# One attention stage, another order: queues of all five engines rearranged within a pair of heads

## The reference

```python
q_bits = (np.einsum('bhsd,dk->bhsk', q, proj) > 0)      # the same for k; 6 bits give a bucket
mask = q_bucket[:, :, :, None] == k_bucket[:, :, None, :]
scores = np.where(mask, scale * np.matmul(q, k.transpose(0, 1, 3, 2)), -1000000000.0)
attn = np.exp(scores - np.max(scores, axis=-1, keepdims=True))
attn = attn / (np.sum(attn, axis=-1, keepdims=True) + 1e-09)
x = np.matmul(attn, v)                                   # reshaped to 1536 x 512
...
h = np.maximum(x @ w_in, 0.0)                            # 512 x 2048
x = h * h @ w_out                                        # 2048 x 512
...
h = np.maximum(x[mask] @ w1[e], 0.0)                     # 8 experts, 192 tokens each
out[mask] = h @ w2[e]
```

## Time and profile before

| | us |
|---|---|
| median of 3 runs | 838.34 (834.74 to 838.97) |
| profiled execution, its own time | 838.97 |
| its span in the trace | 837.2 |
| PE busy over the span | 783.4 (94%) |
| ACT, DVE, POOL busy | 377.2, 379.8, 398.9 |

### The profile page before, as it was taken

How to read it: one execution, slowest core, us unless ns; L and a number is a source line. 1 busy time by engine, 2 the same in 40 slices (tenths; PEclk the granted TensorE clock), 3 DMA queues, 4 the chain that set the end, 5 groups by cost and what they waited for, 6 DMA issues and landing times. The chain is left out here.

```text
span 837.2 us, 14217 instructions
## 1 busy us (share of the span) xinstructions
PE 783.4 (94%) x4720; PEld 714.6 (85%) x4720; DVE 379.8 (45%) x875; ACT 377.2 (45%) x655; POOL 398.9 (48%) x326
## 2 busy tenths in 40 slices
PE   5999999999999799999999999984599999999986
PEld 3898898898887688999999999973499999999986
DVE  6576576576672443322232234224555345345500
ACT  2677777777676455545545554530012122212221
POOL 5567777777577576646656675640100110011001
PEclk9999999999999899999999999995599999999999
DMA  6564775875541000100000010010635455364541
GB/s 157 121 150 109 157 180 127 187 187 126 141 126 51 0 1 0 38 1 0 1 38 0 0 39 0 0 38 0 220 122 173 166 176 183 119 218 149 179 170 38
DMA packets 43687, 81.38 MB, mean 97 GB/s; under 512 B 17176, under 2 KB 17176, under 8 KB 43136
## 3 DMA queue, kind: packets, MB, share of 16 engines
q1 hardware_dynamic: 41440, 74.58, 31.5%
q0 software_dynamic: 2048, 6.29, 2.3%
q10 hardware_dynamic: 160, 0.00, 0.0%
HBM read 54.55 MB, written 6.29 MB: 73 GB/s over the span
## 5 line engine op out<-in xcount | busy, mean ns | idle before, releaser
L1122 PE MATMUL banks<-xt_hi,split_parts 128*128 128x384 f32 (+1 forms) x512 | 142.2, 339 | 0.2 <-POOL split_parts L886 0.2
L309 POOL TENSOR_TENSOR pt_lo<-pt,pt_hi 128x768 fp32r<-128x768 f32 x64 | 117.7, 1846 | 48.0 <-ACT pt_hi L438 38.4
L1133 PE MATMUL banks<-split_parts,h_hi 128*128 128x512 f32 x384 | 122.8, 401 | 5.7 <-DVE h_lo L1048 5.6
L886 POOL TENSOR_TENSOR split_parts<-w_in_sb,split_parts 128x512 fp32r<-128x512 f32 x64 | 84.4, 1319 | 91.1 <-ACT split_parts L879 89.8
L1045 DVE TENSOR_TENSOR h<-relu 128x384 f32<-128x384 f32 x64 | 43.6, 681 | 184.6 <-ACT relu L1000 184.6
L431 ACT ACTIVATE pt<-banks 128x768 f32<-128x768 f32 x96 | 78.1, 813 | 60.8 <-PE banks L683 54.2
L544 DVE TENSOR_REDUCE mx<-banks 128x1 f32<-128x768 f32 x96 | 90.5, 957 | 23.4 <-PE banks L710 19.5
L1566 PE MATMUL banks<-x_cols,w_in_sb 128*128 128x192 f32 x512 | 96.6, 342 | 1.1 <-ACT x_cols L1346 1.1
L1122 PEld LDWEIGHTS banks<-xt_hi,split_parts 128*128 128x128 f32 x512 | 94.3, 190 | 3.3 <-POOL split_parts L886 0.5
L1580 PE MATMUL banks<-expert_hidden,w_out_sb 128*128 128x192 f32 x512 | 94.0, 334 | 0.0
L890 POOL TENSOR_TENSOR split_parts<-w_out_sb,split_parts 128x512 fp32r<-128x512 f32 x64 | 84.2, 1315 | 16.2 <-ACT split_parts L882 16.2
(11 more groups left out here) (195 smaller groups left out, 1354.6 us busy)
## 6 DMA issues: line engine op xcount, KB each, us to landing
w_in_sb<-in_moe_w SPq DMA_DIRECT2D x8, 2048.0 KB, 9.7
w_out_sb<-in_moe_w SPq DMA_DIRECT2D x8, 2048.0 KB, 8.6
w_in_sb<-in_moe_w_in SPq DMA_DIRECT2D x8, 512.0 KB, 6.5
w_out_sb<-in_moe_w_out SPq DMA_DIRECT2D x8, 512.0 KB, 6.4
w_out_sb<-in_k SPq DMA_DIRECT2D x16, 192.0 KB, 3.7
w_out_sb<-in_q SPq DMA_DIRECT2D x16, 192.0 KB, 4.0
v_raw<-in_v SPq DMA_DIRECT2D x16, 192.0 KB, 3.4
ka<-split_parts SPq DMA_DIRECT2D x16, 192.0 KB, 3.0
```

Source lines behind the costliest of these rows:

```text
L309: pool.tensor_tensor(pt_lo[x % 2][:], pt[j % 2][:], pt_hi[x % 2][:].bitcast(fp32), ALU.subtract).then_inc(los, 1)
L886: pool.tensor_tensor(wil[i], in_view(f), wih[i].bitcast(fp32), ALU.subtract).then_inc(wils, 1)
L1122: last = pe.matmul(PB[i][:, 0:HALF], w_[:, k, :], x_[:, xs], start=n == 0, stop=n == 3 * DT - 1)
L1133: last = pe.matmul(PB[2 + t][:], h_[:, tc], w_[:], start=start and n == 0, stop=stop and n == 2, skip_group_check=True)
```

## The change

No instruction is added or removed. Within a pair the lists of all engines are written in another order:

- PE: a pair begins with `z_k` and tile 0, then `weigh_low(2p - 1, 4)` and `weigh(2p - 1, 5)`, then tile 1 and `z_q`. In the odd head tile 0 comes before `weigh_low(2p, 4)`, tile 1 before the first two score tiles of the next head, and `weigh_low(2p + 1, 1)` before tile 4. Some `fallback`, `weigh_high` and `weigh_low` change places.
- ACT: `high(p - 1)` moves up to just behind `expo(2p, 0)`, `k_high` moves down behind `expo_high(2p, 1)`, `q_high` up ahead of `row`, `v_high` down behind `row` and `v_sum_high`.
- POOL: `low(p - 1)` and `k_low(p + 2)` exchange places.
- DVE: `k_bits` before `q_bits`, `max_done` before `sum_v` or the last `row_max` before `sum_v`.
- SP: `free_row(2p - 1)` first; both `weights` and `more_q` move into the second half of the pair.

```diff
--- before.py
+++ after.py
@@ -244,24 +244,25 @@
             more_k(2)
             more_q(2)
             for p in range(PAIRS):
+                if p:
+                    free_row(2 * p - 1, 1)
                 asm_kb(2 * p + 1, 1)
                 part_ka(1, p % 2)
-                if p:
-                    free_row(2 * p - 1, 1)
                 asm_qb(2 * p + 1, 1)
                 if p:
                     load_v(2 * p + 1, 1)
-                weights(2 * p)
                 part_qa(1, p % 2)
-                weights(2 * p + 1)
                 if p + 1 < PAIRS:
                     asm_kb(2 * p + 2, 0)
                     asm_qb(2 * p + 2, 0)
                     free_row(2 * p, 0)
+                more_q(p + 3)
+                weights(2 * p)
+                if p + 1 < PAIRS:
+                    load_v(2 * p + 2, 0)
                     part_ka(0, (p + 1) % 2)
-                    load_v(2 * p + 2, 0)
                 more_k(p + 3)
-                more_q(p + 3)
+                weights(2 * p + 1)
                 if p + 1 < PAIRS:
                     part_qa(0, (p + 1) % 2)
             for loaded in (ka_in, kb_in, qa_in, qb_in):
@@ -346,8 +347,8 @@
             k_low(pool, 1)
             q_low(pool, 1)
             for p in range(PAIRS):
-                if p + 2 < PAIRS:
-                    k_low(pool, p + 2)
+                if p:
+                    low(p - 1)
                 low_part(2 * p, 1)
                 low_part(2 * p, 2)
                 low_part(2 * p, 3)
@@ -355,8 +356,7 @@
                 v_low_part(2 * p + 1, 1)
                 if p + 2 < PAIRS:
                     q_low(pool, p + 2)
-                if p:
-                    low(p - 1)
+                    k_low(pool, p + 2)
                 low_part(2 * p + 1, 1)
                 low_part(2 * p + 1, 2)
                 low_part(2 * p + 1, 3)
@@ -466,10 +466,11 @@
             v_sum_high(0)
             for p in range(PAIRS):
                 expo(2 * p, 0)
+                high(p - 1)
                 sums(2 * p - 1, 1)
-                k_high(p + 2)
                 expo(2 * p, 1)
                 expo_high(2 * p, 1)
+                k_high(p + 2)
                 expo(2 * p, 2)
                 expo_high(2 * p, 2)
                 expo(2 * p, 3)
@@ -484,13 +485,12 @@
                     split["in_high"](act, 0, 0)
                     split["in_high"](act, 1, 1)
                     split["out_high"](act, 0, 0)
-                v_high(2 * p + 1, 1)
                 expo_high(2 * p, 4)
                 expo(2 * p, 5)
-                high(p - 1)
+                q_high(p + 2)
                 row(2 * p + 1, 1)
-                q_high(p + 2)
                 v_sum_high(2 * p + 1)
+                v_high(2 * p + 1, 1)
                 expo(2 * p + 1, 0)
                 sums(2 * p, 0)
                 expo(2 * p + 1, 1)
@@ -502,9 +502,9 @@
                 expo(2 * p + 1, 4)
                 expo_high(2 * p + 1, 4)
                 expo(2 * p + 1, 5)
+                v_sum_high(2 * p + 2)
                 row(2 * p + 2, 0)
                 v_high(2 * p + 2, 0)
-                v_sum_high(2 * p + 2)
             sums(HEADS - 1, 1)
             high(PAIRS - 1)
 
@@ -593,15 +593,15 @@
                     turn(2 * p - 1, 1, 0)
                     turn(2 * p - 1, 1, 1)
                 if not last:
+                    k_bits(p + 1, kbit[w]).then_inc(kbits, 1)
                     q_bits(p + 1, qbit[w]).then_inc(qbits, 1)
-                    k_bits(p + 1, kbit[w]).then_inc(kbits, 1)
                 row_max(2 * p + 1, 0)
                 row_max(2 * p + 1, 1)
                 row_max(2 * p + 1, 2)
                 row_max(2 * p + 1, 3)
                 row_max(2 * p + 1, 4)
+                row_max(2 * p + 1, 5)
                 sum_v(2 * p + 1, 1)
-                row_max(2 * p + 1, 5)
                 max_done(2 * p + 1)
                 v_low(2 * p + 1, 1)
                 turn(2 * p, 0, 0)
@@ -613,8 +613,8 @@
                     row_max(2 * p + 2, 3)
                     row_max(2 * p + 2, 4)
                     row_max(2 * p + 2, 5)
+                    max_done(2 * p + 2)
                     sum_v(2 * p + 2, 0)
-                    max_done(2 * p + 2)
                 invert(p)
                 if not last:
                     v_low(2 * p + 2, 0)
@@ -761,15 +761,15 @@
 
             def pair(p, w, first, last):
 
-                if not first:
-                    weigh(2 * p - 1, 1, 5)
+                if not last:
+                    z_k(p + 1, w)
                 scores_t(2 * p, 0, p, 0)
                 if not first:
-                    weigh_low(2 * p - 1, 1, 4, False, True)
+                    weigh_low(2 * p - 1, 1, 4)
+                    weigh(2 * p - 1, 1, 5, False, True)
+                scores_t(2 * p, 0, p, 1)
                 if not last:
                     z_q(p + 1, w)
-                    z_k(p + 1, w)
-                scores_t(2 * p, 0, p, 1)
                 weigh(2 * p, 0, 0, True)
                 scores(2 * p + 1, 1, p, 0, None if last else p + 1)
                 scores_t(2 * p, 0, p, 2)
@@ -777,11 +777,11 @@
                 weigh_high(2 * p, 0, 1)
                 scores(2 * p + 1, 1, p, 2, None if last else p + 1)
                 scores_t(2 * p, 0, p, 3)
+                fallback(2 * p, 0, 0)
                 scores(2 * p + 1, 1, p, 3, None if last else p + 1)
-                fallback(2 * p, 0, 0)
                 weigh_low(2 * p, 0, 1)
+                fallback(2 * p, 0, 1)
                 scores(2 * p + 1, 1, p, 4, None if last else p + 1)
-                fallback(2 * p, 0, 1)
                 scores_t(2 * p, 0, p, 4)
                 scores(2 * p + 1, 1, p, 5, None if last else p + 1)
                 weigh_high(2 * p, 0, 2)
@@ -791,13 +791,13 @@
                 weigh_low(2 * p, 0, 3)
                 rows(2 * p + 1, 1)
                 weigh(2 * p, 0, 5)
+                scores_t(2 * p + 1, 1, p, 0)
                 weigh_low(2 * p, 0, 4)
-                scores_t(2 * p + 1, 1, p, 0)
                 weigh_high(2 * p, 0, 4, False, True)
+                scores_t(2 * p + 1, 1, p, 1)
                 if not last:
                     scores(2 * p + 2, 0, p + 1, 0, None)
                     scores(2 * p + 2, 0, p + 1, 1, None)
-                scores_t(2 * p + 1, 1, p, 1)
                 weigh(2 * p + 1, 1, 0, True)
                 scores_t(2 * p + 1, 1, p, 2)
                 if not last:
@@ -811,17 +811,17 @@
                 weigh_high(2 * p + 1, 1, 2)
                 if not last:
                     scores(2 * p + 2, 0, p + 1, 5, None)
+                weigh_low(2 * p + 1, 1, 1)
+                scores_t(2 * p + 1, 1, p, 4)
                 fallback(2 * p + 1, 1, 0)
-                scores_t(2 * p + 1, 1, p, 4)
-                weigh_low(2 * p + 1, 1, 1)
+                weigh_high(2 * p + 1, 1, 3)
                 weigh_low(2 * p + 1, 1, 2)
                 fallback(2 * p + 1, 1, 1)
-                weigh_high(2 * p + 1, 1, 3)
                 scores_t(2 * p + 1, 1, p, 5)
                 if not last:
                     rows(2 * p + 2, 0)
+                weigh_low(2 * p + 1, 1, 3)
                 weigh_high(2 * p + 1, 1, 4)
-                weigh_low(2 * p + 1, 1, 3)
 
             pe.wait_ge(proj_split, 1)
 
@@ -835,8 +835,8 @@
                 pair(p, 0, False, False)
                 pair(p + 1, 1, False, False)
             pair(PAIRS - 1, 0, False, True)
-            weigh(HEADS - 1, 1, 5)
-            weigh_low(HEADS - 1, 1, 4, False, True)
+            weigh_low(HEADS - 1, 1, 4)
+            weigh(HEADS - 1, 1, 5, False, True)
 
 
 def routing_constants(nc, ctx):
```

## The result

| | before | after |
|---|---|---|
| median of the runs on the same chip | 836.75 (834.74 to 838.97) | 865.95 (862.17 to 868.55) |
| profiled execution, its own time | 838.97 | 864.65 |
| its span | 837.2 | 862.9 |

What follows compares the result with a forecast made beforehand. PE was taken to set the pace in the steady pairs, with real losses at the ends. Terms +1.0 - 0.5 + 4.3 + 5.95 + 2.5 - 1.2 = +12.05 us took the median from 838.34 to 850.4, range 844.5 to 856.5.

Steps and rivals of the forecast that it cites:

- SP's queue: Steady pairs: transfers issued together bring `qa` late for PE's first tile, 2.9 us in pair 4; +4.3 us, bounds 0 and 8.
- More is late: Rival: 200 GB/s or the burst delaying copies behind it, 8 us instead of 4.3, start's upper end; 855 to 856, chance 0.15.
- The burst that fits: Rival: SP's burst of transfers is in time, all other terms hold; 846 us, chance 0.18.
- the clock that holds: Rival: clock stays up through the last pair's wait and rises in time at the start; 846.7 us, chance 0.07.
- both forms of an ACT wait already met: Rivals, last pair: `qa` lands before ACT needs it; burst fits, 836, chance 0.04; burst late or wait halved, 840 to 842, 0.06.
- Last pair: Pair 7: ACT's `high(6)` waits for the last `qa` transfer, delaying PE's `weigh(14, 0)`; +5.95 us, bounds 5.5 and 6.3.
- The clock after it: Last pair: PE's granted clock falls to about half after its 6.7 us idle; +2.5 us, bounds 1.5 and 3.
- End of attention: Head 15: `weigh_low(15, 1)` before tile 4 frees POOL's low parts earlier; -1.2 us, bounds -1.6 and -0.7.
- Start: Start of attention: a new PE idle near 24.3 to 25.4 may delay the clock's rise; +1.0 us, bounds -0.2 and +2.1.
- Steady pairs: PE's order in the steady pairs: the small stalls between instructions vanish; -0.5 us, bounds -0.5 to 0.

Runs made afterwards that it cites:

- kernel with both queues mended: Changed kernel with SP's list of before and with `high(6)` and `low(6)` alone at their old places; measured 837.83 us, ratio 1.000.
- the kernel with the guard: Changed kernel with `high(6)` and `low(6)`, and nothing else, at their old places; measured 858.85 us, ratio 1.024.

## Why the prediction was wrong, step by step

Direction, places and the two large mechanisms came out as written; the term for SP's queue was mis-sized, 4.3 us where it and the clock behind it cost 17.7.

**SP's queue: the step that failed.** The text put +4.3 us here, bounds 0 and 8. Measured: 13.0 us of PE's idle before four tiles and 4.7 of slow clock behind three of them, 17.7. Its upper bound was added up wrongly, too: at 200 GB/s the text's own terms give 5.5 for pair 4's burst, 2.95 each for those of pairs 2 and 3 and 2.4 for pair 5's, 13.8 and not 8. (Pair 5's 3.15 MB are 3.08 by shapes, which changes little.) With 13.8 the measured waits would have been inside the bound, by luck, since the rate was not 200. Most inputs were right. The burst's first load was put 19.6 us behind zero; it was issued at 103.78 - 84.22 = 19.56. The burst was put at 11.9 us of bytes at 237 GB/s; it moved at 228, which makes 12.4. PE wanted the tile at 119.89 - 3.53 = 116.36, and 116.07 was forecast. What was missing stands at the end. By mean rate pair 2's burst is over at 104.9 + 12.4 = 117.3. The slowest of the 16 DMA engines came to the end of `qa`, read from the small transfer queued behind it, at 118.78, 1.5 later (the first one at 116.93), and PE's tile started 1.1 behind that, at 119.89. Pair 4: 177.1 + 14.85 (3.34 MB at 225 GB/s) = 191.95, the slowest engine at 193.71, PE at 194.78. So the step "at 237 the last of it is there at 180.9" took the moment at which the mean rate has moved the bytes for the moment at which PE may start; between the two lie, in pairs 2 and 4, 1.5 to 1.8 us for the slowest engine and 1.1 for the landing, and 0.5 to 0.8 for the lower rate. In all the tile started 3.1, 2.8 and 3.6 us later than 237 GB/s would have had the bytes moved, in the bursts of pairs 2, 3 and 4.

Part of that could have been read before. In the last pair of the kernel before, v and the two halves of `qa`, 576 KB, are issued last, from 241.67 on the earlier trace rows:

```profile
241.67 0.60 SPq L172 DMA_DIRECT2D v_raw<-in_v  x1
242.32 0.64 SPq L186 DMA_DIRECT2D qa<-xt_hi  x1
```

With 1.1 us to the first byte and 2.5 for 576 KB at 237 GB/s they would be over at 245.3. The last landed at 246.7 to 246.8, 1.5 later. The text used that landing for ACT and not for PE. The Trainium skill, "DMA: Bandwidth & Descriptors", section "Why a DMA increments its semaphore by 16 and not by 1", says that a DMA's engines finish independently and that only the full count of 16 means the data has landed; this trace agrees, with 1.85 us between the first and the last engine behind pair 2's burst.

**The clock behind the stalls** was in no term for the steady pairs: 4.7 us. I counted slow clock behind 5.6 and 6.7 us of idle and not behind 2.9. With stalls of 0.7 there would have been none, so this error is a child of the first.

**More is late**, the rival with 855 to 856 and 0.15, was nearest, and too small by its own sum: it had 8 us from a rate of 200 GB/s, where 200 gives up to 13.8. The rate was 225 to 228, and the rest was the burst's end. The burst that fits, the clock that holds and both forms of an ACT wait already met are refuted by the rows above.

**Last pair, +5.95: right.** PE's idle before the f32 weigh is 6.79 instead of 0.55 before the tile, +6.2, bounds 5.5 and 6.3. ACT's idle is 6.53, ended by `qa`, 6.3 said. **The clock after it, +2.5: right**, half of 5.15 is 2.6.

**End of attention, -1.2: the right way, and somewhat too large.** From the weigh of head 14 to L1133 were 279.54 - 242.59 = 36.95 us before and 306.51 - 267.85 = 38.66 after; without 2.6 for the clock 36.1, so -0.9. The four kernels that have this order and no slow clock there took 36.4 to 36.8, so -0.1 to -0.6, short of the bound of -0.7.

**Start, +1.0: wrong, about 0.** The first projection of pair 1 stands at 53.38, against 55.86 - 2.34 = 53.52. The gap of 0.90 us at 24.73 is there, but the clock rose at 23.8, not after 28. In the other kernels with this start it rose at 22.3 to 29.0, and the projection stood at 53.1 to 54.5. So the order doesn't set that moment as I had assumed; about 1 us of the start differs from run to run.

**Steady pairs, -0.5: wrong, 0 or a small loss.** The kernel with both queues mended takes 30.78 to 30.86 us for each of pairs 1 to 4, like before, and 31.62 for pair 5, 0.7 more. The small gain that I let PE's order have isn't there.

**The sum.** Start -0.1; pairs 1 to 5 take 172.70 instead of 154.35, +18.35, of which 12.4 is the waits for `qa`, 4.7 the clock and 1.2 something else; pair 6's tile 0.6; last pair 6.2 and 2.6; end -0.9: +26.8 of the +27.0 at the mark. The 1.2 lie in pairs 3 and 4. About half of them, 0.15 and 0.42 us, is idle of PE that ends with DVE's `v_sum_c`; the kernel before has no such idle there. The rest stays open.

```profile
149.47 0.52 PE L719 MATMUL banks<-identr,mn 128*3 128x128 f32 x6 [0.15 <-DVE v_sum_c L560]
...
185.90 0.52 PE L719 MATMUL banks<-identr,mn 128*3 128x128 f32 x6 [0.42 <-DVE v_sum_c L560]
```

## What to carry to other kernels

When many transfers are put back to back on one queue, ask when the slowest DMA engine has finished the last of them, and add the landing; bytes by mean rate gives too early a time, here by 2.8 to 3.6 us. A few us of TensorE's idle can cost more than themselves: count the slow clock behind each. And a copy that is moved forward in an engine's list takes its waits with it: look at every instance for one that waits for something else than its siblings (here `high(6)`, the seventh), and guard that one alone.

## What the runs showed of the hardware

- SP's queue moved 225 to 228 GB/s over 14 to 17 us in the bursts of the change, with all 16 DMA engines busy, mostly in packets of 256 B to 8 KB. The rate is not one number: with the same list it was 245 GB/s in the kernel before and 212 with `high` moved, from 182 to 194.
- Behind the bursts of pairs 2 to 4 the 16 engines ended 1.7 to 2.2 us apart in the change, 0.6 to 1.3 behind the same bursts in the kernel with the guard, and up to 3.5 with SP's list alone (187.02 and 190.50 behind pair 4's burst); in the shorter or earlier bursts 0.2 to 1.9. With `part_qa(0)` moved ahead it was 1.4 to 2.5. In the kernel before, the same small transfer has 0.1 to 0.2 throughout.
- Half clock came behind idles of PE of 2.3, 2.5, 2.8, 3.1 us and the longer ones, and not behind 1.9, 2.0 and, in two kernels, 2.5 and 3.0 us. The stretches behind idles of up to 3.5 us lasted 3.4 us, those behind idles of 4 to 7 us 3.4 to 10.2, most of them 6.8. I had not expected it behind so short idles: the three of 12.4 us together cost 4.7 us more.
- A stretch of half clock can begin inside the idle (191.1, with the work starting at 194.78), so that part of it costs nothing: 1.6 us were lost in 6.8.
